# A fused attention and mixture-of-experts kernel: the chosen expert's second weights split in two halves around the state rows, part of expert 0's low parts made on GpSimd, its second load issued later

## The chip, the core and the metric

The kernel is one program on one core of a Trainium2 chip. The metric is the device time of a run in microseconds (us); the kernel before ran three times, 1128.51 to 1131.19 us, median 1130.11 us. Engines are named as in the profile: PE is TensorE, ACT is ScalarE, DVE is VectorE, POOL is GpSimd, SP is SyncE, which here only issues DMAs.

## What is computed

Three stages follow one another. Only the third, and the passage into it, is touched.

```python
xread, sread = two attentions between x (8 x 8 x 512 x 64) and state (8 x 8 x 32 x 64)
x = [xread, sread] as rows                     # 8 x 544 = 4352 rows of 512
h = x @ w_in; x = (h * clip(h + 3, 0, 6) / 6) @ w_out        # 512 -> 2048 -> 512
logits = x @ w_gate; e_idx = argmax(logits)    # 8 experts
for e in range(8):
    h  = max(x[e_idx == e] @ w1[e], 0)         # 512 -> 1024
    ye = h @ w2[e]                             # 1024 -> 512
    out[e_idx == e] = gate_w * sigmoid(x @ w_output_gate)[e] * ye
```

## The kernel before

Every product is made from two parts of each operand, a high part in fp32r (a copy made by ACT) and a low part (the operand less its high part, made by DVE), as three matmuls: high by high, high by low, low by high.

**The blocks.** Attention and the first MLP run over eight blocks of 512 rows, and then over one block B of the 256 state rows. After each block its rows are routed: the logits, the chosen expert, the place of each row among its expert's rows. POOL scatters the rows to `buckets` in HBM (`scatter_rows`, L757).

**The tiles of the expert stage.** The rows of an expert are worked in tiles of 128. Of tile t, `first` (L1014) multiplies the turned rows by the expert's first weights in two halves of 512 columns, `relu` (L1245, ACT) evicts a half, `hidden_out` (L656, SP) writes it to HBM and `hidden_back` (L663) reads it back in another layout, `turn_hidden` (L1626, DVE) and `hidden_hi` / `hidden_lo` (L1237 ACT, L1633 DVE) turn and split it, `second` (L1038) multiplies it by the second weights, `put_out` (L1616, DVE) scales it, and POOL scatters it to the output (L789). The rows of a tile come by `load_rows` (L640), `turn_rows` (L1604, DVE), `rows_hi` (L1218, ACT) and `rows_lo` (L1594, DVE).

**The weights.** An expert's first weights (2 MB) are loaded to `raw1`, the second weights (2 MB) to `raw2`, or for the first two experts to `raw2_first0` and `raw2_first1`. `split_hi` (L1210, ACT) and `split_lo` (L564, DVE) make high and low parts in four pieces of 128 x 1024. `w1_ready` and `w2_ready` count experts whose parts are all made; PE waits for them.

**The passage (PRE = 3 tiles).** After block 7 the fullest expert so far is chosen (`star`), and its first three tiles are worked while the state rows are still being routed. PE's order after the first MLP is: tile 0 first half, transposes of state rows 0 (`side(B + 1, 0)`), tile 0 second half, logits of state rows 0 and transposes 1, tile 1 first half, logits 1, tile 1 second half, tile 2 first half, ranks, tile 2 second half, the count of rows of all experts (L1052), then `second` of tiles 0, 1 and 2. From tile 3 on (expert 0, whose parts lie in the other weight slot) the order is `first(t)`, `second(t - 3)`.

**The table.** Meanwhile DVE computes from the counts which rows, expert and weight slot each of the 41 tiles has: a chain of small operations on 128 x 41 or 128 x 328 elements, each waiting for the one in front of it, from L1663 to L1749, with `turn_hidden`, `hidden_lo`, `put_out` and `turn_rows` of tiles 0 to 4 in between. `table_rows_ready` after L1688 lets SP load tile 3's rows; `order_ready` after L1722 is waited for by PE behind `first` of tile 3; `table_ready` after L1749 is waited for by ACT ahead of `relu` of tile 3 and by SP and POOL.

ACT, DVE, POOL and SP run what they are given in written order, so a wait holds whatever is written behind it on the same engine.

Of the kernel before, what the change touches and what calls it, by code (L numbers as in the profile page):

```python
# [29 lines left out]
ALU = mybir.AluOpType  # L30
# [9 lines left out]
def emit_kernel(nc, x_rows, x_t_dram, keys, w_in, w_out, gates, w1, w2, out):  # L40
# [30 lines left out]
    PRE = 3  # L71
# [144 lines left out]
    MT = MAX_TILES  # L216
# [90 lines left out]
    def sem(name):  # L307
        if name not in sems:
            sems[name] = nc.alloc_semaphore(name)
        return sems[name]  # L310
# [57 lines left out]
    def is_b(b, n):  # L368
        return isinstance(b, int) and b == n
# [164 lines left out]
    def by_pieces(raw):  # L534

        return raw[:].rearrange("p (i c) -> p i c", i=w1.shape[1])
# [38 lines left out]
    def _(sp):  # L575
# [134 lines left out]
        sp.wait_ge(sem("second_ready"), 1)  # L710
        e = sp.value_load(table[0:1, T_NEXT, MT:MT + 1], min_val=0, max_val=E - 1)
        sp.wait_ge(sem("w1_ready"), 2)
        sp.dma_start(by_pieces(raw1), w1[bass.ds(e, 1)].rearrange("o i p c -> p (o i) c")).then_inc(sem("raw1_loaded"), 16)
        load_rows(Tile(0, PRE + 2))

# [16 lines left out]
    def _(pool):  # L732
# [19 lines left out]
        def scatter_rows(b, tiles):  # L752

            wait(pool, "place_ready", b + 1)
            pool.sem_inc(sem("scatter_begun"), 1)
            for t in range(tiles):
                pool.indirect_dma_start(out=buckets, out_offset=bass.IndirectOffsetOnAxis(ap=place[:, t:t + 1], axis=0),  # L757
                                        in_=rows_of(b)[:, t, :], in_offset=None,
                                        bounds_check=limit, oob_is_err=False
                                        ).then_inc(sem("rows_stored"), 16)  # L760
# [18 lines left out]

        pool.wait_ge(sem("pads_stored"), 16 * (E + 1))  # L780

        scatter_rows(B, ST)

        def body(t):

            slot = t.slot
            wait(pool, "out_ready", t.n + 1)
            pool.sem_inc(sem("store_begun"), 1)
            pool.indirect_dma_start(out=out, out_offset=bass.IndirectOffsetOnAxis(ap=out_row[:, slot:slot + 1], axis=0),  # L789
                                    in_=yo_of(t)[:], in_offset=None, bounds_check=last_row, oob_is_err=False  # L790
                                    ).then_inc(sem(f"out_stored{slot}"), 16)

        for n in range(PRE):
            body(Tile(0, n))
        pool.wait_ge(sem("table_ready"), 1)
        stored = [pool.value_load(stores[0:1, s:s + 1], min_val=16 * (N_TOK // P // RING), max_val=16 * MT)
                  for s in range(RING)]
# [8 lines left out]
    def _(pe):  # L806
# [212 lines left out]
        def first(t):  # L1019

            expert, w_at = weights(t)
            wait(pe, "w1_ready", expert + 1)
            wait(pe, "xg_t_ready", t.n + 1)
            for h in range(HALVES):
                first_half(t, h, w_at)
# [46 lines left out]
    def _(act):  # L1072
# [167 lines left out]
        def relu(t, h):  # L1240
            wait(act, "hid2_ps", HALVES * t.n + h + 1)

            if h == 0:
                wait(act, "hid_written", 16 * HALVES * t.n)
            act.activation(expert_hid_of(t)[:, h * BANK:h * BANK + BANK], hid2_banks[t.slot % 2][:, h, :], ACT.Relu  # L1245
                           ).then_inc(sem("act_ready"), 1)

        side(B + 1, 0)
        relu(Tile(0, 0), 0)
        split_hi(1, 0, 0)  # L1250

        act.dma_start(by_pieces(raw2_first[1]), w2[0].rearrange("i p c -> p i c")).then_inc(sem("raw2_loaded"), 16)
        relu(Tile(0, 0), 1)
        side(B + 1, 1)
        rows_hi(Tile(0, 2))
        split_hi(0, 1, WSLOT, (0, 1))
        relu(Tile(0, 1), 0)
        side(B + 1, 2)
        split_hi(0, 1, WSLOT, (2, 3))
        relu(Tile(0, 1), 1)  # L1260
        hidden_hi(Tile(0, 0))
        relu(Tile(0, 2), 0)
        relu(Tile(0, 2), 1)
        hidden_hi(Tile(0, 1))
        split_hi(1, 1, WSLOT)
        hidden_hi(Tile(0, 2))
        rows_hi(Tile(0, 3))
        rows_hi(Tile(0, 4))
        act.wait_ge(sem("table_ready"), 1)
        act.wait_ge(sem("pads_stored"), 16 * (E + 1))  # L1270
# [53 lines left out]
    def _(dve):  # L1324
# [319 lines left out]
            mlp_block(b, S, CH)  # L1644
        mlp_block(B, NSB, ST)

        split_lo(dve, 1, 0, 0, signal="w2_ready")
        turn_rows(Tile(0, 2))
        side(B + 1, 1)
        rows_lo(Tile(0, 2))  # L1650
        split_lo(dve, 0, 1, WSLOT, (0, 1))
        side(B + 1, 2)
        split_lo(dve, 0, 1, WSLOT, (2, 3), "w1_ready")
        turn_hidden(Tile(0, 0))
        side(B + 1, 4)
        hidden_lo(Tile(0, 0))

        dve.wait_ge(sem("iota2"), 5)
        chain(dve.tensor_scalar(upto[:], upto[:], 0.0, None, ALU.is_ge))
        chain(dve.memset(t_chg[:, MT - 1:MT], 0.0))  # L1660
        dve.wait_ge(sem("count_ps"), 2)

        chain(dve.tensor_tensor(count[:], b_ps[:, 0, 0:E], star_sub[:], ALU.subtract))  # L1663
# [96 lines left out]
        def body(t):  # L1760
            split1 = split_code(dve, t)
            two_back = not (isinstance(t.n, int) and t.n < PRE + 2)
            if two_back:
                split2 = split_code(dve, t.plus(-2))
            split_first(t, split1)
            if not (isinstance(t.n, int) and t.n + 2 >= MT):
                turn_rows(t.plus(2))
                rows_lo(t.plus(2))
            if is_b(t.n, PRE):
                split_lo(dve, 1, 1, WSLOT, signal="w2_ready")  # L1770
            if two_back:
                with dve.If(split2 > 0):
                    split_lo(dve, 1, *next_of(split2), signal="w2_ready")
            if not is_b(t.n, PRE):
                turn_hidden(t.plus(-1))
                hidden_lo(t.plus(-1))
                if not (isinstance(t.n, int) and t.n < PRE + LAG2):
                    put_out(t.plus(-LAG2))
# [60 lines left out]
```

## Time and profile before

| | |
|---|---|
| runs | 1128.51, 1130.11, 1131.19 us |
| profiled execution | 1128.17 us, its span 1126.4 us |
| PE busy | 1104.0 us of the span, 6199 matmuls |
| DVE, ACT, POOL busy | 658.5, 476.6, 74.7 us |
| first MLP ends on PE | 685.2 us |
| tiles 0 to 2 on PE | 685.2 to 727.2 us |
| last result | 1126.4 us |

The span is the time from the first to the last instruction, 1.8 us less than the execution's own time. PE's busy time counts matmuls that overlap as one; what is left of the span is time in which PE had nothing that it was allowed to run.

### The profile page before, as it was taken

Reading aid. Unit: us, or ns where it says so; the run is one execution under the profiler, and the core shown is the slowest. Engines: PE = TensorE matmul, PEld = TensorE weight load, DVE = VectorE, ACT = ScalarE, POOL = GpSimd, SP = SyncE. Lnnn points to the kernel's source line nnn. Section 1 sums busy time; section 2 is a strip of 40 time slices with the busy share of each in tenths; the row PEclk is TensorE's granted clock in tenths of the full one; section 3 lists DMA queues with packets and bytes.
Section 4 is the critical chain, followed back from the end, with each engine's and each line's share of the span. In section 5 each row is a group of like instructions: output and inputs, shape, how many; then the busy total and the mean of one; then the engine's idle time right before and its main releaser. Section 6 shows DMA issues by size and latency. Waiting matters only on the chain.

```text
span 1126.4 us, 20220 instructions
## 1 busy us (share of the span) xinstructions
PE 1104.0 (98%) x6199; PEld 872.0 (77%) x6200; DVE 658.5 (58%) x1269; ACT 476.6 (42%) x789; POOL 74.7 (7%) x95
## 2 busy tenths in 40 slices
PE   9999999999999999999999999899999999999996
PEld 7777777777777777777777988677888888878885
DVE  6674665655655646646555455875665645558632
ACT  4454434434443443444354445343444333435320
POOL 0000100100101001001001010100011110101011
PEclk9999999999999999999999999999999999999999
DMA  9210211111102102111004079659877654785541
GB/s 364 106 39 1 76 39 38 38 39 38 43 33 75 38 1 76 38 38 40 1 1 132 1 260 285 197 174 284 263 240 232 218 173 139 234 258 181 168 154 60
DMA packets 129794, 135.59 MB, mean 120 GB/s; under 512 B 13999, under 2 KB 107823, under 8 KB 127152
## 3 DMA queue, kind: packets, MB, share of 16 engines
q1 hardware_dynamic: 95056, 87.26, 24.9%
q10 hardware_dynamic: 28896, 29.36, 8.3%
q0 software_dynamic: 5760, 17.90, 4.3%
q8 instruction: 49, 0.80, 0.3%
q14 instruction: 33, 0.27, 0.1%
HBM read 90.06 MB, written 45.47 MB: 120 GB/s over the span
## 4 chain that ended last, share of the span: by engine, by line
PE 87%; DVE 5%; DMA 2%; ACT 2%; issue 2%; SPq 1%; ACTq 1%; DVEq 0%; POOL 0%; POOLq 0%
PE y_ps L964 34%; PE h_ps L946 16%; PE y_ps L1038 15%; PE h_ps L1014 7%; PE y_ps L1014 6%; PE a_ps L921 3%; PE h_ps L936 2%; DMA hid_mv<-hidden 1%; DVE we L564 1%; ACT we L1210 1%; PE a_ps L819 1%; PE a_ps L905 1%; SPq L663 1%; PE a_ps L885 1%; PE b_ps L827 1%
## 5 line engine op out<-in xcount | busy, mean ns | idle before, releaser
L964 PE MATMUL y_ps<-w_out_hi,hid_hi 128*128 128x512 f32 x512 | 204.7, 400 | 0.0
L964 PE MATMUL y_ps<-w_out_hi,hid_lo 128*128 128x512 f32 x512 | 199.7, 390 | 0.0
L964 PE MATMUL y_ps<-w_out_lo,hid_hi 128*128 128x512 f32 x512 | 199.4, 389 | 0.0
L1038 PE MATMUL y_ps<-we,act_t_hi 128*128 (+1 forms) x608 | 188.5, 391 | 4.2 <-DVE yo L1616 2.2
L946 PE MATMUL h_ps<-att_hi,mix 128*128 128x512 f32 x512 | 184.1, 402 | 0.1
L1550 DVE SCALAR_TENSOR_TENSOR hid<-hid,h_ps 128x512 f32<-128x512 f32 x128 | 87.7, 685 | 144.9 <-ACT hid L1159 144.9
L1159 ACT ACTIVATE hid<-h_ps,three 128x512 f32<-128x512 f32 x128 | 87.9, 687 | 150.5 <-PE h_ps L946 150.4
L1038 PEld LDWEIGHTS y_ps<-we,act_t_hi 128*128 128x128 f32 x608 | 114.6, 189 | 28.9 <-issue 5.3
L964 PEld LDWEIGHTS y_ps<-w_out_hi,hid_hi 128*128 128x128 f32 x512 | 96.0, 188 | 49.1 <-issue 30.4
L1558 DVE TENSOR_TENSOR hid_lo<-hid,hid_hi 128x512 fp32r<-128x512 f32 x128 | 88.0, 687 | 62.8 <-ACT hid_hi L1166 62.3
L1038 PE MATMUL y_ps<-we,act_t_lo 128*128 (+1 forms) x304 | 118.7, 391 | 0.0
L946 PEld LDWEIGHTS h_ps<-att_hi,mix 128*128 128x128 f32 x512 | 96.1, 188 | 27.4 <-issue 7.0
L964 PEld LDWEIGHTS y_ps<-w_out_hi,hid_lo 128*128 128x128 f32 x512 | 96.1, 188 | 20.9
L964 PEld LDWEIGHTS y_ps<-w_out_lo,hid_hi 128*128 128x128 f32 x512 | 96.2, 188 | 18.8
L1166 ACT ACTIVATE hid_hi<-hid 128x512 fp32r<-128x512 f32 x128 | 80.7, 631 | 62.2 <-DVE hid L1550 59.9
L1237 ACT ACTIVATE act_t_hi<-act_raw 128x512 fp32r<-128x512 f32 x76 | 46.5, 632 | 129.2 <-DVE act_raw L1626 129.2
L946 PE MATMUL h_ps<-att_lo,mix 128*128 128x512 f32 x256 | 99.9, 390 | 0.0
L1014 PE MATMUL h_ps<-we,xg_t_hi 128*128 (+1 forms) x304 | 94.0, 390 | 2.5 <-DVE we L564 1.7
L1014 PE MATMUL y_ps<-we,xg_t_hi 128*128 (+1 forms) x304 | 94.1, 391 | 1.1 <-DVE xg_t_lo L1594 1.1
L1626 DVE STREAM_TRANSPOSE act_raw<-hid_mv 128x512 f32<-128x512 f32 x74 | 48.2, 689 | 60.4 <-DMA hid_mv<-hidden 30.6
L564 DVE TENSOR_TENSOR we<-raw,we 128x1024 f32 (+1 forms) x56 | 65.1, 1221 | 20.5 <-ACT we L1210 20.5
L757 POOL DMA_INDIRECT buckets<-rows,place x32 | 31.9, 998 | 594.9 <-DVE place L1496 587.6
(251 smaller groups left out, 1511.7 us busy)
## 6 DMA issues: line engine op xcount, KB each, us to landing
raw<-in_w ACTq DMA_DIRECT2D x12, 2048.0 KB, 10.6
hid_mv<-hidden SPq DMA_DIRECT2D x148, 128.0 KB
hidden<-expert_hid SPq DMA_DIRECT2D x70, 256.0 KB
xg<-buckets SPq DMA_DIRECT2D x156, 64.0 KB
xb<-in_x_rows SPq DMA_DIRECT2D x8, 1024.0 KB, 4.8
x_t<-in_x_t SPq DMA_DIRECT2D x7, 1024.0 KB, 4.9
buckets<-pad_row SPq DMA_DIRECT2D x8, 774.0 KB, 8.0
w_in_raw<-in_w_in SPq DMA_DIRECT2D x4, 1024.0 KB, 13.5
```

The lines of the kernel that those rows point to most:

```text
L564: ins = eng.tensor_tensor(we[:, bass.ds(w_at + piece(w, i, LO), PIECE)], raw[:, i * PIECE:(i + 1) * PIECE], we[:, bass.ds(w_at + piece(w, ...
L921: i = pe.matmul(mix_bank(a, n, g)[NS * q:NS * q + NS, :], keys_of(a)[D * g:D * g + D, q, :], w_in_raw[D * g:D * g + D, q, mix_columns(n)], ...
L946: i = pe.matmul(h_ps[:, j % 2, 0:cols], mix[:, m % SLOTS, g, n % GO, wp, :], (att1_hi, att1_lo)[tp][:, g, 0:cols], start=(g == 0 and k == ...
L964: i = pe.matmul(y_ps[:, t, :], hid_of(b, j)[1 + hp][:, t * P:(t + 1) * P], w_out_s[wp][:, j, :], start=(j == 0 and m == 0), stop=(j == KF ...
L1014: i = pe.matmul(hid2_banks[slot % 2][:, h, :], xg_t[xp][:, slot % 2, k, :], we[:, bass.ds(w_at + (wp * WPART + k * F + h * BANK), BANK)], ...
L1038: i = pe.matmul(y2_ps[:, slot % 2, :], act_t[hp][:, slot % 2, f, :], we[:, bass.ds(w_at + (wp * WPART + KD * F + f * DM), DM)], start=(f = ...
L1159: act.activation(whole, h_ps[:, j % 2, 0:cols], ACT.Relu, bias=three).then_inc(sem("relu_ready"), 1)
L1166: act.activation(high, whole, ACT.Copy).then_inc(sem("hid_hi_ready"), 1)
L1237: act.activation(act_t[HI][:, slot % 2, h * 4:h * 4 + 4, :], act_raw[:, slot % 2, h * 4:h * 4 + 4, :], ACT.Copy).then_inc(sem("act_t_hi"), 1)
L1550: dve.scalar_tensor_tensor(out=whole, in0=whole, scalar=6.0, in1=h_ps[:, j % 2, 0:cols], op0=ALU.min, op1=ALU.mult).then_inc(sem("swish_re ...
L1558: dve.tensor_tensor(low, whole, high.bitcast(F32), ALU.subtract).then_inc(sem("hid_ready"), 1)
L1626: dve.transpose(act_raw[:, slot % 2, h * 4:h * 4 + 4, :].rearrange("p f t -> p (f t)"), hid_mv_of(t)[:, h, :, :].rearrange("p s (k f) -> p ...
```

## The change

- ACT copies pieces 0 and 1 of the chosen expert's second weights ahead of the copy of the transposed state rows, and pieces 2 and 3 behind the first half's `relu` of tile 0; before, all four stood behind that `relu`.
- ACT issues the load of expert 0's second weights (`raw2_first1`, 2 MB) behind `relu` of tile 2; before, ahead of the second `relu` of tile 0.
- Pieces 2 and 3 of expert 0's first weights get their low parts from POOL (signal `w1_lo_pool`); PE waits for it ahead of tile 3, SP ahead of the next load into `raw1`.
- All four pieces of expert 0's second weights get their low parts from POOL, around its output scatters of tiles 0 to 2; before, DVE made them in tile 3's turn.
- ACT makes the high parts of these second weights in two halves around `rows_hi` of tile 3, behind `hidden_hi` of tile 2; before, all four ahead of `hidden_hi` of tile 2.
- DVE does two small operations of the table (`upto`, `t_chg`) before the passage. ACT does the second `relu` of tile 1 ahead of the last two `split_hi` pieces.

```diff
@@ sync, ahead of the load of the next first weights @@
         sp.wait_ge(sem("w1_ready"), 2)
+        sp.wait_ge(sem("w1_lo_pool"), 1)
@@ gpsimd @@
+        split_lo(pool, 0, 1, WSLOT, (2, 3), "w1_lo_pool")
         scatter_rows(B, ST)
...
-        for n in range(PRE):
-            body(Tile(0, n))
+        body(Tile(0, 0))
+        split_lo(pool, 1, 1, WSLOT, (0, 1, 2))
+        body(Tile(0, 1))
+        split_lo(pool, 1, 1, WSLOT, (3,), "w2_ready")
+        body(Tile(0, 2))
@@ tensor, first(t) @@
             wait(pe, "w1_ready", expert + 1)
+            if is_b(t.n, PRE):
+                pe.wait_ge(sem("w1_lo_pool"), 1)
@@ scalar @@
+        split_hi(1, 0, 0, (0, 1))
         side(B + 1, 0)
         relu(Tile(0, 0), 0)
-        split_hi(1, 0, 0)
-
-        act.dma_start(by_pieces(raw2_first[1]), w2[0].rearrange("i p c -> p i c")).then_inc(sem("raw2_loaded"), 16)
+        split_hi(1, 0, 0, (2, 3))
         relu(Tile(0, 0), 1)
         side(B + 1, 1)
         rows_hi(Tile(0, 2))
         split_hi(0, 1, WSLOT, (0, 1))
         relu(Tile(0, 1), 0)
         side(B + 1, 2)
+        relu(Tile(0, 1), 1)
         split_hi(0, 1, WSLOT, (2, 3))
-        relu(Tile(0, 1), 1)
         hidden_hi(Tile(0, 0))
         relu(Tile(0, 2), 0)
         relu(Tile(0, 2), 1)
+
+        act.dma_start(by_pieces(raw2_first[1]), w2[0].rearrange("i p c -> p i c")).then_inc(sem("raw2_loaded"), 16)
         hidden_hi(Tile(0, 1))
-        split_hi(1, 1, WSLOT)
         hidden_hi(Tile(0, 2))
+        split_hi(1, 1, WSLOT, (0, 1))
         rows_hi(Tile(0, 3))
+        split_hi(1, 1, WSLOT, (2, 3))
         rows_hi(Tile(0, 4))
@@ vector @@
+        dve.wait_ge(sem("iota2"), 5)
+        chain(dve.tensor_scalar(upto[:], upto[:], 0.0, None, ALU.is_ge))
+        chain(dve.memset(t_chg[:, MT - 1:MT], 0.0))
         split_lo(dve, 1, 0, 0, signal="w2_ready")
         turn_rows(Tile(0, 2))
         side(B + 1, 1)
         rows_lo(Tile(0, 2))
-        split_lo(dve, 0, 1, WSLOT, (0, 1))
+        split_lo(dve, 0, 1, WSLOT, (0, 1), "w1_ready")
         side(B + 1, 2)
-        split_lo(dve, 0, 1, WSLOT, (2, 3), "w1_ready")
...
-        dve.wait_ge(sem("iota2"), 5)
-        chain(dve.tensor_scalar(upto[:], upto[:], 0.0, None, ALU.is_ge))
-        chain(dve.memset(t_chg[:, MT - 1:MT], 0.0))
@@ vector, body(t) @@
-            if is_b(t.n, PRE):
-                split_lo(dve, 1, 1, WSLOT, signal="w2_ready")
```

What stands on POOL between its last constant and the wait for the table, before. `rows_state` are the 256 state rows, `yo` and `yo_pre` the results of tiles 0 to 2.

```order
L778 IOTA slot_back 128x4
L757 DMA buckets<-rows_state,place 38016x516 [waits pads_stored,place_ready]
L757 DMA buckets<-rows_state,place 38016x516
L789 DMA out<-yo_169,out_row 4352x512 [waits out_ready]
L789 DMA out<-yo_pre,out_row 4352x512 [waits out_ready]
L789 DMA out<-yo_169,out_row 4352x512 [waits out_ready]
```

The same place of the changed kernel. `raw_164` are expert 0's first weights, `raw_first_149` its second.

```order
L779 IOTA slot_back 128x4
L564 TENSOR_TENSOR we<-raw_164,we 128x1024 [waits w1_hi,pads_stored]
L564 TENSOR_TENSOR we<-raw_164,we 128x1024 [waits w1_hi]
L758 DMA buckets<-rows_state,place 38016x516 [waits place_ready]
L758 DMA buckets<-rows_state,place 38016x516
L792 DMA out<-yo_169,out_row 4352x512 [waits out_ready]
L564 TENSOR_TENSOR we<-raw_first_149,we 128x1024 [waits w2_hi] x3
L792 DMA out<-yo_pre,out_row 4352x512 [waits out_ready]
L564 TENSOR_TENSOR we<-raw_first_149,we 128x1024 [waits w2_hi]
L792 DMA out<-yo_169,out_row 4352x512 [waits out_ready]
```

Six subtractions with two inputs in SBUF now stand among POOL's scatters.

ACT at the beginning of the passage, before. `raw_first_148` are the chosen expert's second weights.

```order
L1180 ACTIVATE rows_state<-y_ps 128x512 [waits y_ps] x2
L1079 ACTIVATE rows_state_t<-a_ps 128x512 [waits t_ps]
L1245 ACTIVATE expert_hid_pre<-h_ps 128x512 [waits hid2_ps]
L1210 ACTIVATE we<-raw_first_148 128x1024 [waits raw2_loaded]
L1210 ACTIVATE we<-raw_first_148 128x1024 x3
L1252 DMA raw_first_149<-in_w 128x16x256
L1245 ACTIVATE expert_hid_pre<-h_ps 128x512 [waits hid2_ps]
```

The same place of the changed kernel.

```order
L1188 ACTIVATE rows_state<-y_ps 128x512 [waits y_ps] x2
L1218 ACTIVATE we<-raw_first_148 128x1024 [waits raw2_loaded]
L1218 ACTIVATE we<-raw_first_148 128x1024
L1087 ACTIVATE rows_state_t<-a_ps 128x512 [waits t_ps]
L1253 ACTIVATE expert_hid_pre<-h_ps 128x512 [waits hid2_ps]
L1218 ACTIVATE we<-raw_first_148 128x1024 [waits raw2_loaded]
L1218 ACTIVATE we<-raw_first_148 128x1024
L1253 ACTIVATE expert_hid_pre<-h_ps 128x512 [waits hid2_ps]
```

Two copies moved ahead of the transposed state rows, and the load left this place.

## Rows read from the trace of the kernel before

**Rows 1.** The page: busy time by engine.
```profile
PE 1104.0 (98%) x6199; PEld 872.0 (77%) x6200; DVE 658.5 (58%) x1269; ACT 476.6 (42%) x789; POOL 74.7 (7%) x95
```
**Rows 2.** PE's waits from 684 to 800 us: us, times, longest.
```profile
PE y_ps L1038 <- DVE yo L1616: 2.2, 1, 2.2
PE b_ps L1052 <- DVE seen L1499: 1.6, 1, 1.6
PE y_ps L1038 <- DVE act_t_lo L1633: 1.1, 1, 1.1
PE y_ps L1014 <- DVE xg_t_lo L1594: 1.1, 1, 1.1
PE h_ps L1014 <- issue: 0.9, 1, 0.9
PE y_ps L1038 <- issue: 0.8, 1, 0.8
PE b_ps L849 <- DVE logits L1331: 0.6, 1, 0.6
```
**Rows 3.** PE's timeline: start, us, instruction, idle before it; the count, tiles 0 and 7.
```profile
707.17 0.18 PE L1052 MATMUL b_ps<-seen,ones 128*128 128x8 bf16 x1 [1.63 <-DVE seen L1499]
708.46 1.19 PE L1038 MATMUL y_ps<-we,act_t_hi 128*128 128x512 f32 x2 [1.11 <-DVE act_t_lo L1633]
...
757.04 0.73 PE L1014 MATMUL y_ps<-we,xg_t_hi 128*128 x2 [1.05 <-DVE xg_t_lo L1594]
```
**Rows 4.** Windows: us, PE, PEld, DVE, ACT, POOL busy, granted PE clock, DMA.
```profile
708.00:710.00 2.00, 1.54 (x4) 1.28 (x5) 1.76 (x8) 0.00 (x0) 1.70 (x2) 0.50 0.69 198
```
**Rows 5.** ACT's timeline in the passage.
```profile
688.53 0.60 ACT L1079 ACTIVATE rows_state_t<-a_ps 128x512 f32<-128x512 f32 x1 [2.56 <-PE a_ps L819]
...
689.50 3.90 ACT L1210 ACTIVATE we<-raw_first 128x1024 fp32r<-128x1024 f32 x4
693.30 0.59 ACT L1245 ACTIVATE expert_hid_pre<-h_ps 128x512 f32<-128x512 f32 x1
```
**Rows 6.** SP's timeline: the hidden layer of tiles 0 and 2, out and back.
```profile
699.63 2.67 SPq L663 DMA_DIRECT2D hid_mv<-hidden  x4
...
708.69 1.01 SPq L656 DMA_DIRECT2D hidden<-expert_hid_pre  x2
713.57 2.53 SPq L663 DMA_DIRECT2D hid_mv<-hidden  x4
```
**Rows 7.** DMA queues from 693 to 699 us, ACT's: packets, MB, share of 16 engines.
```profile
q10 hardware_dynamic: 1538, 1.56, 78.2%
```
**Rows 8.** DVE's timeline from tile 2's hidden layer on.
```profile
718.97 1.31 DVE L1626 STREAM_TRANSPOSE act_raw<-hid_mv 128x512 f32<-128x512 f32 x2 [0.67 <-DMA hid_mv<-hidden]
...
734.26 0.18 DVE L1749 CAST table<-t_next 128x41 int32<-128x41 f32 x1
...
737.97 4.62 DVE L564 TENSOR_TENSOR we<-raw_first,we 128x1024 fp32r<-128x1024 f32 x4
...
745.98 1.30 DVE L1626 STREAM_TRANSPOSE act_raw<-hid_mv 128x512 f32<-128x512 f32 x2 [1.37 <-DMA hid_mv<-hidden]
...
769.66 1.30 DVE L1626 STREAM_TRANSPOSE act_raw<-hid_mv 128x512 f32<-128x512 f32 x2 [5.83 <-DMA hid_mv<-hidden]
```
**Rows 9.** The chain of waits: the write of tile 1's hidden layer: start, us, what.
```profile
704.02 2.01 DMA hidden<-expert_hid_pre
```
**Rows 10.** POOL's groups by shape: the only operation that reads SBUF elementwise.
```profile
L738 POOL TENSOR_SCALAR_AFFINE_SELECT ident<-ident 128x128 f32<-128x128 f32 x1 | 0.3, 288 | 0.3 <-POOL three L735 0.3
```
**Rows 11.** POOL's timeline: the two longest of its 72 scatters, and one beside them.
```profile
595.53 1.39 POOL L757 DMA_INDIRECT buckets<-rows,place  x1 [0.30 <-issue]
597.23 0.97 POOL L757 DMA_INDIRECT buckets<-rows,place  x1 [0.30 <-issue]
...
707.66 1.51 POOL L757 DMA_INDIRECT buckets<-rows_state,place  x1 [49.94 <-DVE place L1496]
```
**Rows 12.** A read-back of the hidden layer beside two loads of weights: its issue.
```profile
758.28 3.00 SPq L663 DMA_DIRECT2D hid_mv<-hidden  x4
```

## The prediction

> **What bounds it.** I read the page first: PE is busy for 1104.0 of 1126.4 us [rows 1]. The change adds and removes no matmul, so its reach is PE's 22 us without one. The table of PE's waits says where those lie that it can touch: 8.3 us in seven waits between 684 and 800 us, two behind results of the passage (`seen`, tile 0's `act_t_lo`), one behind tile 2's hidden layer (0.8), the others behind tiles 5 to 8 [rows 2]. To the first two a price belongs that no wait shows: from 708 to 710 us the granted clock is 0.50, the 1.2 GHz level, after PE had idled for 1.6 and 1.1 us with one small matmul between [rows 3, 4]. The first pair there takes 1.19 us [rows 3], the same pair 0.73 at the upper level [rows 3]; over the nine matmuls until the clock is back I estimate 1.4 us.
>
> Then I followed the other engines' timelines to see what sets the end of the stretch. Three things in a row do. (a) The hidden layers of tiles 0 to 2 go to HBM and back one after the other on SP; tile 2's is back at 718.97, DVE having waited 0.67 for it [rows 6, 8]. (b) From there DVE is never idle for long until the last table entry ends at 734.44, 15.5 us later [rows 8]. (c) ACT's `relu` of tile 3 waits for that table; tile 3's hidden layer is back at 745.98 [rows 8], behind it ACT and DVE split the next first weights, behind those stand tile 7's rows, and PE starts tile 7 at 757.04 [rows 3], 22.6 us behind the table. PE's waits of 1.1 and 2.2 us [rows 2] lie at the end of this sequence, not on matmuls. So **what counts is when the table is ready**; PE will idle until that plus 22.6 us whatever it gained earlier.
>
> **Part by part.** The sum is made against the profiled execution (span 1126.4, own time 1128.17 us), which is 1.9 us under the median 1130.11; I carry differences over unchanged.
>
> 1. Second weights in halves. ACT idled 2.56 us ahead of the state rows' copy [rows 5]; two of four copies at 0.98 us fit there, if the load has landed. On ACT's queue three loads of 2.1 MB pass from 676 to 699 us, 1.56 MB of them in its last 6 us [rows 7]; counting backwards the first is complete at about 685.4. The second `relu` of tile 0 then starts at 691.5 instead of 693.30 [rows 5], 1.8 us earlier. PE's 0.6 us wait for the logits goes too, since DVE's four subtractions end at 693 instead of 695.2.
>
> 2. The load leaves the queue. Behind the `relu` of 693.30 the read-back was issued only at 699.63 [rows 5, 6], 5.7 us after it ended, while ACT's queue moved its last 1.56 MB [rows 7]; for tile 1, with nothing beside it, it took 2.0 us [rows 9]. With the load gone I take 2.0: the read-back of tile 0 at 694.3, 5.3 us earlier, and tile 1's some 4 us earlier, near 702.3, set by PE's own pace.
>
> 3. Tile 2's hidden layer. PE ends tile 2 at 705.5 before [rows 3], at 704.7 now; its `relu` follows at once and SP is free: written from 705.2 instead of 708.69 [rows 6]. Now the moved load starts beside it (issue about 705.3), with the state rows' scatter. Undisturbed, the read-back would be in at 713.8; disturbed as the one issued at 758.28 [rows 12], which DVE got at 769.66 [rows 8] (11.4 us, where tile 2's took 5.4), at 720. A load of 2 MB beside it instead of the two there gives a third of that: 716.7, a gain of 2.3 us on 718.97 (ends: 5.2 and -1). DVE could not have used it before 714.6.
>
> 4. DVE's part of the first weights (two pieces, 2.3 us) leaves the passage. Tile 0's hidden layer is turned from 700.3, over 4 us earlier, ranks are placed by 702.8; without hindrance PE would go on from tile 2 to the count and tile 0's `second` at 704.8 instead of 708.46 [rows 3], at full clock. That is worth 3.7 + 1.4 us at that point, and nothing at the end, since PE then waits for tile 2 (716.7 + 2.7) and for (c).
>
> 5. `upto` and `t_chg` moved: 0.35 us off DVE, in front of a wait. Nothing.
>
> 6. DVE's 4.62 us of second weights at 737.97 [rows 8] go. Tile 6's rows are ready earlier and PE's 0.9 us wait [rows 2] disappears, but DVE had waited for tile 3's hidden layer at 745.98 anyway, so PE takes the 0.9 us again at tile 7. Nothing at the end.
>
> 7. What POOL does instead. No row shows a subtraction on POOL. From below: DVE's own 1.16 us a piece. The nearest row is the select of 128x128, 288 ns [rows 10], with one input: 2.25 ns a column, 2.3 us for 1024 columns; with every input costing that, 4.6. I take 2.3. Six pieces are 14 us on an engine that is 7% busy [rows 1]. The first two run from 701.2 to 705.8; the state rows' scatter behind them starts then, not later than 707.66 before [rows 11]. Three run behind the scatter of tile 0, from 720, when ACT has made their high parts (now behind tile 2's `hidden_hi`), one behind tile 1's. PE needs them at about 750, SP's added wait is over 15 us before its load, PE's added wait likewise. The output scatters of tiles 1 and 2 come later; nobody waits for them before 757. If POOL and DVE leave each other alone, all of it costs nothing.
>
> 8. **What POOL's subtractions do to DVE.** Two scatters of 72 are clearly longer than 0.97 us: 1.39 and 1.51, each while DVE ran a string of small operations in SBUF [rows 11]: 0.4 and 0.5 us of holding off, once each. Nothing shows the other direction with a POOL operation that reads two inputs. Bounds: none, or the whole of each piece in which DVE next meets an operation with two SBUF inputs (`rows_lo`, `used_no` at L1698, `over_mt` at L1714 and most steps of the table are such). With whole pieces: the piece at 720.0 holds `used_no` from 720.65 to 722.3 (1.65); the next takes hold as soon as that ends, 2.25; the third meets `over_mt` (0.75) and the fourth tile 4's `rows_lo` (0.9): 5.5 us between 718 and the last table entry. In the passage the first pair delays `seen` to 706.3 and tile 0's low part to 707.5, so that most of step 4 stays as it was, the low clock too. I take the whole: POOL's work is a piece at a time with no gap, and the string of table steps meets it everywhere.
>
> The Trainium skill, "SBUF — State Buffer", section "Who interferes with whom", says that a VectorE instruction with two SBUF inputs and a GpSimd one that reads SBUF exclude each other, the later one being fully blocked. By it step 8 is 5.5 us; by the scatters' 0.4 to 0.5 us a time four meetings would be 2. For the piece, "GPSIMD Engine Reference", section 3.1, has 4497 ns for 2048 columns; an estimate from it is 2.25 us.
>
> **Sum.** Table ready: -2.3 (step 3) + 5.5 (step 8) = +3.2 us, and from there the 22.6 us as before: 1130.1 + 3.2 = **1133.3 us**.
>
> **Rivals.**
> - *No holding off*: step 8 is nothing, the table is 2.3 to 3 us earlier, PE idles some 3 us ahead of tile 2's `second` and then follows. 1127.4 us, faster. For it: DVE's and POOL's other work beside each other shows 0.5 us at the most. Against: none of that work reads two inputs on POOL.
> - *Half of it*: holding off as in the scatters, or pieces that fall into DVE's one-input work (transposes, reductions); 2 to 2.5 us eat the gain of step 3. 1130.1 us, no change.
> - *The load collides*: no holding off, but tile 2's read-back is as slow as behind two loads, at 720 or later. The table is then 1 us later than before: 1131 us, at 722 slower by 3. It decides from 719 on.
> - *The halves don't fit*: if the first load lands after 687 us, `relu` of tile 0 and the state rows' copy slip by as much; each is covered by steps 2 and 3 up to 2 us. No case of its own.
>
> **Numbers.** A run of this kernel can tell 0.2%, 2.3 us, from no change. Whole holding off 0.44: slower 0.40, same 0.04. None 0.30: faster 0.24, same 0.06. Half 0.16: faster 0.04, same 0.10, slower 0.02. Collision 0.10: same 0.07, slower 0.03. So faster 0.28, same 0.27, slower 0.45. The likeliest case alone spans 1131.3 to 1135.5 (pieces of 1.7 to 3 us, step 3 by 1 us either way). Since the other sign has over a quarter, the range reaches from 1126.3 to 1135.5; below lies a gain of the whole 4.3 us that DVE leaves in step 3, above it a piece of 4.6 us.
>
> **What would show it.** Right: POOL's subtractions at 2.3 us or more; DVE's two-input steps of 0.2 us (`used_no`, `upto_n`, `over_mt`) shown as 1 to 2 us or with gaps of that size ahead of them; from tile 2's turned hidden layer to the last table entry 20 to 21 us instead of 15.5; PE's waits ahead of tiles 3, 4, 5 and 7. Read-back of tile 0 issued near 694 (step 2), tile 2's turned near 717 (step 3). Wrong: those 15.5 us unchanged or shorter (then the first rival), or tile 2 turned after 719 (the third). If PE's start of tile 7 moves by another amount than the last table entry does, (c) is wrong, and with it the sum.

## The result, and the profile after

Before and after ran by turns on one chip, five times each: median 1130.62 us before and **1141.13 us after** (1139.10 to 1144.35), ratio 1.0101, 95% interval 1.0083 to 1.0118. (The ratio is estimated from the single runs; the two medians lie 10.5 us apart, 0.9%.) The change costs some 10.5 us, where 3.2 were forecast; 1141.1 lies above the range, which ended at 1135.5. The profiled execution after has a span of 1139.3 us, 12.9 above that of before, whose own time (1128.17) was 2.4 us under its median.

PE of the kernel after, from 684 to 810 us, by what it waited for:

```profile
PE y_ps L1020 <- DVE xg_t_lo L1604: 4.4, 2, 2.8
PE y_ps L1046 <- issue: 3.2, 1, 3.2
PE b_ps L1060 <- DVE seen L1509: 2.5, 1, 2.5
PE y_ps L1046 <- DVE yo L1626: 2.5, 1, 2.5
PE h_ps L1020 <- issue: 1.9, 2, 1.7
PE y_ps L1046 <- DVE act_t_lo L1643: 1.1, 1, 1.1
PE y_ps L1020 <- issue: 0.8, 1, 0.8
```

16.4 us where [rows 2] had 8.3, and none is large: PE waits a little at nearly every tile, as an engine does that follows a late table. The rest of the 12.9 us is busy time: 4.7 us more for the same 6199 matmuls than in [rows 1], and the granted clock is under 1.00 behind some of these waits (the page, then the windows behind the wait of 2.8 us: busy time of PE, its weight load, DVE, ACT, POOL; granted clock, DMA share, GB/s):

```profile
PE 1108.7 (97%) x6199; PEld 875.4 (77%) x6200; DVE 662.9 (58%) x1263; ACT 476.3 (42%) x789; POOL 88.9 (8%) x101
```

```profile
730.00:735.00 5.00, 2.15 (x8) 1.47 (x7) 4.10 (x12) 2.52 (x3) 1.34 (x2) 0.89 0.17 43
735.00:740.00 5.00, 5.00 (x19) 4.00 (x18) 4.86 (x6) 0.63 (x1) 4.83 (x3) 0.77 1.08 361
```

So I follow the table again.

**POOL**, its subtractions and scatters, from 700 to 740 us (start, busy time of the group, how many; the bracket is the idle time ahead):

```profile
703.12 4.71 POOL L564 TENSOR_TENSOR we<-raw,we 128x1024 fp32r<-128x1024 f32 x2 [44.36 <-ACT we L1218]
...
720.98 0.97 POOL L792 DMA_INDIRECT out<-yo,out_row  x1 [9.52 <-DVE yo L1626]
725.65 4.76 POOL L564 TENSOR_TENSOR we<-raw_first,we 128x1024 fp32r<-128x1024 f32 x2 [3.71 <-ACT we L1218]
734.07 2.39 POOL L564 TENSOR_TENSOR we<-raw_first,we 128x1024 fp32r<-128x1024 f32 x1 [3.66 <-ACT we L1218]
736.61 0.99 POOL L792 DMA_INDIRECT out<-yo_pre,out_row  x1
737.62 2.40 POOL L564 TENSOR_TENSOR we<-raw_first,we 128x1024 fp32r<-128x1024 f32 x1
```

A piece takes 2.4 us; step 7 had 2.3. **DVE** beside these pieces (the first two rows from the passage, the rest from the table; the last is the last table entry):

```profile
703.61 1.95 DVE L1495 TENSOR_TENSOR place_f<-place_f,onehot 128x16 f32<-128x16 f32 x1
...
705.80 2.05 DVE L1506 CAST place<-g_best 128x2 int32<-128x2 f32 x1
...
722.65 1.31 DVE L1636 STREAM_TRANSPOSE act_raw<-hid_mv 128x512 f32<-128x512 f32 x2 [2.50 <-DMA hid_mv<-hidden]
...
725.73 2.37 DVE L1704 TENSOR_SCALAR table<-tile_no,total 128x41 int32<-128x41 f32 x1
728.13 2.31 DVE L1706 TENSOR_SCALAR used<-tiles_of 128x8 f32<-128x8 f32 x1
...
735.03 1.45 DVE L1719 TENSOR_SCALAR slot_n<-slot_back,total 128x4 int32<-128x4 f32 x1
...
737.78 2.29 DVE L1726 TENSOR_SCALAR t_left<-t_ord,nth 128x41 f32<-128x41 f32 x1
...
745.50 0.18 DVE L1758 CAST table<-t_next 128x41 int32<-128x41 f32 x1
```

Six operations that take 0.17 to 0.25 us in the kernel before stand for 1.45 to 2.37 us, each until a piece of POOL's ends (725.73 + 2.37 = 728.10, the middle of the pair; 728.13 + 2.31 = 730.44, its end). In the table they add 2.13 + 2.14 + 1.26 + 2.04 = 7.6 us. From tile 2's turned hidden layer (722.65) to the end of the last table entry (745.68) are 23.0 us, where [rows 8] had 15.5.

Its start is late too: 722.65 instead of 718.97 [rows 8]. 1.0 us of that I take as no work of the change: ACT's copy of the state rows, with which the passage begins and up to which the two programs differ by two small operations only (`upto` and `t_chg` on DVE, which then idles for 8.25 us), starts at 685.73 in this execution and at 684.69 in that of before (in the fourteen profiles of this case at 684.47 to 685.76). So 2.6 us are left. **ACT**, then **SP**, then the write of tile 2's hidden layer in the chain of waits (after, and the same of before), then the DMA queues from 706 to 718 us (packets, MB, the time their packets took as a share of 16 engines' span; q10 carries ACT's loads, q1 SP's transfers, q0 POOL's scatters):

```profile
688.82 2.01 ACT L1218 ACTIVATE we<-raw_first 128x1024 fp32r<-128x1024 f32 x2 [1.82 <-DMA raw_first<-in_w]
690.74 0.58 ACT L1087 ACTIVATE rows_state_t<-a_ps 128x512 f32<-128x512 f32 x1
...
693.58 0.60 ACT L1253 ACTIVATE expert_hid_pre<-h_ps 128x512 f32<-128x512 f32 x1
...
705.74 0.39 ACTq L1272 DMA_DIRECT2D raw_first<-in_w  x1
```

```profile
696.24 3.05 SPq L663 DMA_DIRECT2D hid_mv<-hidden  x4
...
706.71 1.21 SPq L656 DMA_DIRECT2D hidden<-expert_hid_pre  x2
717.73 2.54 SPq L663 DMA_DIRECT2D hid_mv<-hidden  x4
```

```profile
707.29 10.42 DMA hidden<-expert_hid_pre
```

```profile
709.27 4.28 DMA hidden<-expert_hid_pre
```

```profile
q10 hardware_dynamic: 2034, 2.07, 58.2%
q1 hardware_dynamic: 1180, 0.95, 26.3%
q0 software_dynamic: 160, 0.53, 11.0%
```

Tile 2's hidden layer is written from 706.71, 2.0 us earlier than before [rows 6], but its read-back is issued only at 717.73, 4.2 us later than before. Its 512 KB went out beside the moved load of 2 MB: the three queues fill 95.5% of those 12 us. It is the write that stood, 10.42 us instead of 4.28. The read-back was in 4.9 us after its issue (722.65), where it had been 5.4.

From the table to tile 7 all is as it was: PE starts tile 7 at 768.20, 22.5 us behind the end of the last table entry, where it had been 22.6. The `second` at 798.18 came at 786.75 before, with a wait of 2.19 instead of 2.48 us; after it the granted clock falls here and did not before. PE of the kernel after, then of before, then windows of the kernel after:

```profile
768.20 0.72 PE L1020 MATMUL y_ps<-we,xg_t_hi 128*128 x2 [1.55 <-DVE xg_t_lo L1604]
...
798.18 0.73 PE L1046 MATMUL y_ps<-we,act_t_hi 128*128 x2 [2.48 <-DVE yo L1626]
```

```profile
786.75 0.72 PE L1038 MATMUL y_ps<-we,act_t_hi 128*128 x2 [2.19 <-DVE yo L1616]
```

```profile
795.00:800.00 5.00, 2.52 (x10) 1.70 (x9) 3.52 (x7) 2.41 (x5) 0.97 (x1) 0.88 0.93 284
800.00:805.00 5.00, 5.00 (x19) 4.00 (x18) 3.92 (x7) 2.56 (x4) 0.00 (x0) 0.78 1.03 346
```

19 matmuls in 5 us instead of 24 at clock 1.00. So the 12.9 us of span are: 1.0 ahead of the passage, tile 2 turned 2.6 later, 7.6 us in the table (together the 11.2 by which tile 7 starts later), 0.3 more ahead of the `second` at 798.18, and an estimated 1.4 us of low clock behind it. Whether that low clock belongs to the change is not shown. Behind the same `second` the clock falls in e2, e6, e8 and e9 below too, and it stays at 1.00 in e4, after a wait of 2.6 us. This term and the 1.0 us at the start vary among the profiled executions whatever the edit, and the two medians lie 2.4 us less apart than the two spans.

### The profile page after: what moved, and what is told of

Read it like the earlier page. It is cut to its first block, busy times and chain, and to the rows that moved or that the text cites. A ratio compares the mean times of both kernels' runs of the same rounds, so it can differ in the third digit from the quotient of the medians.

```text
span 1139.3 us, 20223 instructions
## 1 busy us (share of the span) xinstructions
PE 1108.7 (97%) x6199; PEld 875.4 (77%) x6200; DVE 662.9 (58%) x1263; ACT 476.3 (42%) x789; POOL 88.9 (8%) x101
## 4 chain that ended last, share of the span: by engine, by line
PE 82%; DMA 5%; DVE 5%; issue 2%; ACT 2%; SPq 1%; ACTq 1%; DVEq 0%; POOL 0%; POOLq 0%
PE y_ps L970 32%; PE h_ps L952 16%; PE y_ps L1046 14%; PE h_ps L1020 6%; PE y_ps L1020 6%; PE a_ps L927 3%; DMA raw<-in_w 2%; PE h_ps L942 2%; DMA raw_first<-in_w 1%; DMA hid_mv<-hidden 1%; DVE we L564 1%; DMA hidden<-expert_hid_pre 1%; ACT we L1218 1%; PE a_ps L911 1%; PE a_ps L825 1%
## 5 line engine op out<-in xcount | busy, mean ns | idle before, releaser
L564 DVE TENSOR_TENSOR we<-raw,we 128x1024 f32 (+1 forms) x54 | 62.7, 1222 | 20.6 <-ACT we L1218 20.6
```

The costliest lines, as they stand in the source:

```text
L564: ins = eng.tensor_tensor(we[:, bass.ds(w_at + piece(w, i, LO), PIECE)], raw[:, i * PIECE:(i + 1) * PIECE], we[:, bass.ds(w_at + piece(w, ...
```

## The experiments

Two theories at first. **Both together**: POOL's pieces hold off the table by 7.6 us, the moved load delays tile 2 by 2.6 us, and the sum goes through to the end. **One hidden by the other**: one of the two alone explains the time and the other would be covered. Later ones asked which operations POOL holds off, and whether the load has a place that costs nothing. "Start" is where ACT begins to copy the state rows, "tile 2" how long after it DVE starts to turn tile 2's hidden layer, "table" how long after it the last table entry ends, all in the profiled execution; the stretch lies between the last two. The ratio is the estimate from the single runs, as above; it differs from the quotient of the medians by up to 0.1%.

| kernel | median us (before beside it) | ratio, 95% interval | start | tile 2 | table | stretch |
|---|---|---|---|---|---|---|
| before | 1130.11 |  | 684.69 | 34.3 | 49.8 | 15.5 |
| after | 1141.13 (1130.62) | 1.0101, 1.0083 to 1.0118 | 685.73 | 36.9 | 59.9 | 23.0 |
| e1_load_back | 1134.64 (1129.99) | 1.0047, 1.0030 to 1.0064 | 685.64 | 32.6 | 55.6 | 23.0 |
| e2_no_pool | 1132.88 (1129.99) | 1.0026, 1.0015 to 1.0036 | 684.52 | 37.2 | 52.7 | 15.5 |
| e3_pool_second_only | 1137.39 (1129.99) | 1.0076, 1.0057 to 1.0094 | 685.20 | 34.1 | 58.2 | 24.1 |
| e4_load_only | 1136.01 (1129.99) | 1.0064, 1.0045 to 1.0082 | 684.69 | 40.5 | 55.9 | 15.5 |
| e5_halves_only | 1129.31 (1129.38) | 0.9992, 0.9983 to 1.0001 | 684.47 | 33.9 | 49.4 | 15.5 |
| e6_load_after_tile2 | 1130.38 (1129.38) | 1.0004, 0.9994 to 1.0014 | 684.69 | 31.0 | 50.1 | 19.1 |
| e7_pieces_apart | 1137.20 (1129.38) | 1.0066, 1.0051 to 1.0082 | 685.76 | 33.8 | 57.8 | 24.0 |
| e8_load_after_rows3 | 1133.97 (1130.18) | 1.0032, 1.0021 to 1.0043 | 685.70 | 31.2 | 46.6 | 15.5 |
| e9_rows5_first | 1129.06 (1129.20) | 0.9997, 0.9988 to 1.0006 | 685.24 | 32.1 | 47.6 | 15.5 |
| p2_pool_subtracts, one run | 1132.44 (1129.38) |  | 684.54 | 34.1 | 53.9 | 19.7 |
| p3_pool_memsets, one run | 1127.61 (1130.18) |  | 684.61 | 33.5 | 49.7 | 16.2 |
| p4_pool_copies, one run | 1129.80 (1130.18) |  | 685.37 | 34.1 | 50.5 | 16.4 |

In most of them the time follows the table's column within some 1 us: after +10.2 there and +10.5 in the median, e1 +5.9 and +4.7, e2 +3.0 and +2.9, e3 +8.4 and +7.4, e4 +6.2 and +6.0, e5 -0.3 and -0.1, e6 +0.3 and +1.0, e7 +8.1 and +7.8. In e8 (-3.1 and +3.8) and e9 (-2.1 and -0.1) it does not; there something behind the table is late.

### One part undone

e1_load_back is the kernel after with the load at its old place:

```diff
@@ ACT, before relu(Tile(0, 0), 1)
+        act.dma_start(by_pieces(raw2_first[1]), w2[0].rearrange("i p c -> p i c")).then_inc(sem("raw2_loaded"), 16)
@@ ACT, behind relu(Tile(0, 2), 1)
-        act.dma_start(by_pieces(raw2_first[1]), w2[0].rearrange("i p c -> p i c")).then_inc(sem("raw2_loaded"), 16)
```

> The changed kernel with the load of expert 0's second weights back at its old place, ahead of tile 0's second relu. Theory: two costs add up in the change, the moved load beside tile 2's way through HBM (tile 2's hidden layer was turned at 722.65 instead of 718.97, 3.7 us) and GpSimd's subtractions holding VectorE (7.5 us from there to the last table entry). Then tile 2 is turned near 719, the stretch to the last entry stays about 23 us, and the time is 1141.1 - 3.7 = 1137.4 us. Rival: tile 2 is late because the state rows' scatter stands behind GpSimd's first two pieces; then nothing moves, 1141 us.

Measured 1134.64, 4.65 over its before where after has 10.51: undoing the load's move gives 5.9 us, not the 3.7 expected. Tile 2, and the table with it, come 4.3 us earlier than there, with the state rows' scatter still behind POOL's first two pieces: the rival falls. The other 1.6 us lie behind the table: the `second` that waited 2.48 us at 798.18 waits 0.61 here, and the clock stays at 1.00 behind it (it falls to 0.71 behind tile 7 instead). That they come with the load's place is not shown: e4 has the load moved and takes no longer than before from its table to the end, and each of the two medians is known to some 2 us only.

e2_no_pool is the kernel after with all six pieces made by DVE in their old places; the load and the halves stay moved:

```diff
@@ POOL
-        split_lo(pool, 0, 1, WSLOT, (2, 3), "w1_lo_pool")
...
-        split_lo(pool, 1, 1, WSLOT, (0, 1, 2))
...
-        split_lo(pool, 1, 1, WSLOT, (3,), "w2_ready")
@@ DVE, at the places of before; PE and SP no longer wait for w1_lo_pool
+        split_lo(dve, 0, 1, WSLOT, (2, 3), "w1_ready")
...
+        split_lo(dve, 1, 1, WSLOT, signal="w2_ready")
```

> The changed kernel with all six pieces made on VectorE at the places of the kernel before, no other difference: the load stays moved, the halves stay. Theory: the 7.5 us of held VectorE instructions go, the late tile 2 stays: stretch from tile 2's turn to the last entry 15.5 us, tile 2 near 722, 1141.1 - 7.5 = 1133.6 us. Rival (VectorE is slow in the table for another reason, such as DMA traffic beside it): stretch 23 us, 1141 us or more.

Measured 1132.88, 0.7 under the 1133.6 expected. The stretch is 15.5 us again, and tile 2 is 3.0 us later than before: the load's collision stays, with no piece of POOL's anywhere, and the hold-off is gone.

Do the two parts add? Against e5 below, which has neither, the last table entry is 3.3 us later in e2, 6.2 in e1 and 10.5 with both, 1.0 more than their sum. Over their befores the medians are 2.9 and 4.7 us, and 10.5 with both: 2.9 more than the sum, but each is uncertain by 1 to 2 us. So they add, and whether some 1 to 3 us come on top is not settled.

### One part alone

e3_pool_second_only is the kernel before with the second weights' four pieces on POOL; e4_load_only the kernel before with the load moved; e5_halves_only the kernel after without POOL's pieces and with the load back, so that only ACT's halves and order and DVE's early `upto` remain.

> The kernel before with only the four low parts of expert 0's second weights moved to GpSimd, between its output scatters; ScalarE's order and the load as before. Theory: three or four VectorE instructions of the table are held for up to 2.4 us each, last entry 6 to 8 us later, 1130.6 + 5.5 to 7.5 = 1136 to 1138 us. Rival (holding costs only beside the other edits; the 4.6 us taken off VectorE pay for it): within 1 us of 1130.6.

e3: 1137.39, 7.4 us slower, as expected. POOL's row, then DVE's:

```profile
720.47 6.97 POOL L564 TENSOR_TENSOR we<-raw_first,we 128x1024 fp32r<-128x1024 f32 x3
```

```profile
720.68 7.92 DVE L1636 TENSOR_TENSOR act_t_lo<-act_raw,act_t_hi 128x512 fp32r<-128x512 f32 x2
...
735.51 2.27 DVE L1720 TENSOR_SCALAR t_left<-t_ord,nth 128x41 f32<-128x41 f32 x1
```

The first of the two `act_t_lo` stands 7.3 us, through all three pieces, the second takes its usual 0.68. Tile 2's `second` waits on PE for 7.0 us behind it.

> The kernel before with only the load of expert 0's second weights moved behind tile 2's relu. Theory: the load runs beside tile 1's and tile 2's hidden layers, tile 2 is turned 3 to 4 us later than 718.97 and everything with it: 1130.6 + 3.7 = 1134.3 us. Rival (the load costs nothing at either place, as a read-back issued earlier makes up for it): 1130 us.

e4: 1136.01, 1.7 over the 1134.3 expected. Here ACT's order is the old one, and the load, issued at 706.33, meets tile 1's read-back as well:

```profile
706.04 2.65 SPq L663 DMA_DIRECT2D hid_mv_pre<-hidden  x4
708.80 1.01 SPq L656 DMA_DIRECT2D hidden<-expert_hid_pre  x2
719.86 2.53 SPq L663 DMA_DIRECT2D hid_mv<-hidden  x4
```

```profile
717.82 1.30 DVE L1625 STREAM_TRANSPOSE act_raw<-hid_mv_pre 128x512 f32<-128x512 f32 x2 [7.42 <-DMA hid_mv_pre<-hidden]
```

Again 11 us from the write of tile 2's hidden layer to its read-back; both tiles are late, tile 2 by 6.2 us, and the time follows.

> The kernel before with ScalarE's halves and order and the two early table operations of the change; all pieces on VectorE, the load at its old place. Theory (load and GpSimd are the whole of the loss): tile 0's second relu is 0.5 to 1.8 us earlier but the table is bound by tile 2's hidden layer at about 718.5, so 1129.0 to 1130.0 us, no more than 1 us under the kernel before. Rival (the halves cost by themselves, since ScalarE waits for the first load ahead of the state rows): 1131 to 1132 us.

e5: no difference, as expected. ACT waited 1.8 us for the first load here too, so the halves could not bring all that step 1 wanted.

### What POOL holds off

e7_pieces_apart is e3 with a wait behind each of the first three pieces, so that they don't follow each other at once; p2, p3 and p4 are the kernel before with other work on POOL behind tile 0's scatter, on a buffer that nobody reads any more, with a wait behind each. The three ran once each, so their rows are read and not their times.

```diff
+        ...                      # spare_t: rows_state_t as 128x512
+        for i in range(6):       # p3: 12 x memset; p4: 12 x tensor_copy of 128x256
+            pool.tensor_tensor(spare_t, spare_t, spare_t, ALU.subtract).then_inc(sem("probe"), 1)
+            pool.wait_ge(sem("probe"), i + 1)
```

> The kernel with only expert 0's second weights on GpSimd, with a wait for each of the first three pieces' completion ahead of the next. In the run without the waits one VectorE subtraction of 128x512 stood for 7.3 us, as long as three pieces. Theory (pieces that follow with no gap keep VectorE's two-input instruction out until the last is done): with the gap the instruction gets in between two pieces, lasts 2 to 2.5 us, and the time falls by 2 to 4 us from 1137.4. Rival (a gap makes no difference): 7 us and 1137 us again.

e7: 1137.20, as slow as e3; the 2 to 4 us did not come, though the operation got in between two pieces. The two `act_t_lo` now take 3.11 and 2.82 us instead of 7.32 and 0.68, and next in line a TENSOR_SCALAR of 0.24 stands 2.17: what one operation is spared the next ones pay. A TENSOR_SCALAR of 128x1 between them kept its 0.14 with the third piece running.

> The kernel before with six extra GpSimd subtractions of 128x512 (two inputs in SBUF) behind tile 0's scatter, each waited for; they work on a tile that nobody reads any more. Theory: each is 1.2 us; VectorE's two-input and SBUF-to-SBUF one-input instructions among them stand up to 1.2 us longer, three to five of them; transposes and reductions keep their 0.7 and 0.2 us. Rival: nothing is held by instructions this short.

p2: DVE's `act_t_lo` took 1.48 and 1.52 us, two TENSOR_SCALAR of the table 0.84 and 1.09, `used_no` (two inputs) 0.89; reductions kept their times, as expected. No transpose lay beside these; in the kernel after one that began at 734.41, beside a piece, took its usual 0.70. The stretch grew by 4.3 us.

> The kernel before, with twelve memsets of 128x512 on GpSimd behind the scatter of tile 0's outputs, one after the other with a gap between them (they fill rows_state_t, which nobody reads any more). They write SBUF and read nothing. In p2_pool_subtracts six subtractions of 1.24 us there, with gaps, made tile 2's two act_t_lo 1.48 and 1.52 us long (0.69 alone), two TENSOR_SCALAR of the table 0.84 and 1.09, used_no 0.89. Theory (the Trainium skill's rule, the page SBUF - State Buffer): a two-input VectorE instruction is held off only by a GpSimd instruction that reads SBUF, a one-input one (TENSOR_SCALAR, CAST) by any. By it act_t_lo stay at 0.69 to 0.75 and used_no at 0.2, while some of the TENSOR_SCALAR of 0.14 to 0.2 us (total, table, used) stand at 0.4 us or more. Rival: whatever GpSimd does holds off both sorts; then act_t_lo take 1.0 us or more. Second rival: only GpSimd's two inputs hold anything off; then all stand as in the kernel before.

p3, POOL and then DVE:

```profile
719.90 7.02 POOL L797 MEMSET rows_state_t<- 128x512 f32 x12
```

```profile
719.57 1.29 DVE L1639 TENSOR_TENSOR act_t_lo<-act_raw,act_t_hi 128x512 fp32r<-128x512 f32 x2
...
721.24 0.47 DVE L1701 TENSOR_SCALAR table<-tile_no,total 128x41 int32<-128x41 f32 x1
721.74 0.53 DVE L1703 TENSOR_SCALAR used<-tiles_of 128x8 f32<-128x8 f32 x1
722.31 0.17 DVE L1704 TENSOR_TENSOR used_no<-used,expert_no 128x8 f32<-128x8 f32 x1
```

Beside a writer that reads nothing, both `act_t_lo` and `used_no` keep their times, and TENSOR_SCALAR of 0.24 and 0.17 us stand until a memset of 0.53 ends. The theory's line between the two sorts holds in this execution.

> The same with twelve copies of 128x256 on GpSimd in place of the memsets (one SBUF input, one output). Theory (the skill's rule): both sorts of VectorE instruction are held off, as in p2_pool_subtracts: act_t_lo at 0.9 us or more (0.69 alone) and one or more of the TENSOR_SCALAR of the table and used_no at 0.4 us or more. Rival: only GpSimd instructions with two inputs hold VectorE off; then act_t_lo stay under 0.8 and all small ones under 0.3.

p4: with one input on POOL the two `act_t_lo` take 1.77 us together instead of 1.29, the same two TENSOR_SCALAR 0.38 and 0.41, but `used_no` 0.17 and `upto_n` 0.31. `act_t_lo` is just short of the 0.9 each that was written down; the direction is the theory's, since beside memsets of longer duration they did not move at all. POOL is held too: one of its twelve copies took 0.83 us instead of 0.40.

The Trainium skill, "SBUF — State Buffer", section "Who interferes with whom", says both halves of this: a VectorE instruction with two SBUF inputs contends with a GpSimd instruction that reads SBUF, not with one that only writes it; and a copy, cast or `tensor_scalar` within SBUF can run in a mode that contends with GpSimd. p3 agrees with the first (`act_t_lo` 1.29 us for two beside memsets), and with the second p3 (0.47 and 0.53) and the four TENSOR_SCALAR of the kernel after (1.45 to 2.37 us).

### Where the load could go

All three have DVE make all low parts (e2) and the halves of the chosen expert's weights. The load's place differs, and with it that of expert 0's second high parts; e9 moves tile 5's rows as well.

```diff
@@ e6, ACT: the load behind hidden_hi(Tile(0, 2)), the four high parts behind rows_hi(Tile(0, 4))
@@ e8, ACT: the load one line further down, behind rows_hi(Tile(0, 3))
@@ e9, as e8, and SP
-        load_rows(Tile(0, PRE + 2))      # was behind the load of the next first weights
         sp.wait_ge(sem("second_ready"), 1)
+        load_rows(Tile(0, PRE + 2))      # now ahead of it
@@ e9, ACT: split_hi(1, 1, WSLOT) in tile 3's turn, behind rows_hi of tile 5
```

> As the run without GpSimd's pieces, with the load of expert 0's second weights issued behind tile 2's hidden layer (near 717 us) and its high parts behind tile 4's rows. Theory: no hidden layer of tiles 0 to 2 has a load beside it; tile 2 is turned near 715 to 716 instead of 718.97, the last table entry is 2.5 to 3.5 us earlier than 734.4, 1127 to 1128 us, faster than both kernels. Rival: the load now meets tile 3's rows and the next first weights, ScalarE's four copies stand ahead of tile 3's relu: 1131 us or more.

e6: 1130.38, no difference; the forecast gain did not come, and tile 3's rows, which the rival named, took it, though not to the rival's 1131. Tile 2 is turned at 715.66, 3.3 us earlier than before, so the gain of step 3 exists; DVE does not wait for it there, its own work sets this start. DVE then stands for tile 3's rows:

```profile
715.66 1.29 DVE L1627 STREAM_TRANSPOSE act_raw<-hid_mv 128x512 f32<-128x512 f32 x2
...
723.98 0.71 DVE L1605 STREAM_TRANSPOSE xg_raw<-xg 128x512 f32<-128x512 f32 x1 [3.49 <-DMA xg<-buckets]
```

> e6_load_after_tile2 with one line moved: the load of expert 0's second weights is issued behind tile 3's rows_hi, some 7 us later, instead of behind tile 2's hidden_hi. In e6 the table was late because tile 3's rows came 3.5 us late beside the load, though tile 2 was turned 3.3 us earlier than in the kernel before. Theory (the load costs what it collides with): tile 2 is turned near 715.7 as in e6, tile 3's rows are no longer waited for by more than 0.5 us, the last table entry ends at 731 to 732 instead of 734.4, and the time is 1127 to 1128 us. Rival: the load then runs beside the next first weights and tile 4's rows, and the second weights are ready only after 750; then PE waits for tile 4's rows or the second weights, and the time is 1130 us or more.

e8: 1133.97, 3.8 us slower, where 1127 to 1128 were expected. The table ends 3.1 us earlier than before, counted from the start, as the theory said; then DVE waits 6.1 us for tile 5's rows, which stand behind two loads of 2 MB:

```profile
739.48 0.71 DVE L1605 STREAM_TRANSPOSE xg_raw<-xg 128x512 f32<-128x512 f32 x1 [6.08 <-DMA xg<-buckets]
```

```profile
PE y_ps L1015 <- DVE xg_t_lo L1595: 6.0, 1, 6.0
```

> e8_load_after_rows3 with two things moved: SP issues tile 5's rows ahead of the next first weights instead of behind them, and ACT makes expert 0's second high parts behind tile 3's relu and tile 5's rows_hi instead of ahead of them. In e8 the last table entry ended at 732.3, 2.3 us earlier than in the kernel before, but two loads of 2 MB lay in front of tile 5's rows, DVE waited 6.1 us for them at 739.5 and PE as much at 742.2; and ACT's split waited 10.2 us for its load with tile 3's relu behind it. Theory (each load costs what stands behind it): the last table entry again at 732 to 733, tile 5's rows turned at 734 or before, tile 7 started by PE at 755 to 756 instead of 757.04, and the time 1127.5 to 1129 us, a little under the kernel before. Rival: with two loads in the air until 736 or later the second weights are split too late, or tile 3's hidden layer is as slow beside them as tile 2's was in the changed kernel (10 us for its write); then PE starts tile 7 at 757 or later and the time is 1130 us or more.

e9: 1129.06, no difference. The table ends 2.1 us earlier, but tile 3's hidden layer is turned at 746.42 (745.98 before) and PE starts tile 7 at 757.48 (757.04 before; 755 to 756 expected): counted from the start both are where they were, and the 2.1 us are gone. None of the three places gave a gain, and no version here beats the kernel before.

## Why the prediction was wrong

Its sign came out and one of its two mechanisms (slower was the likeliest case, by POOL holding off DVE); what it said of tile 2's way through HBM did not, and so the size did not: +3.2 forecast, +10.5 measured. Of the 7.3 us between them step 3 has 4.9 and step 8 has 2.1.

- **Step 1, failed.** "Counting backwards the first is complete at about 685.4": ACT still waited 1.82 us for it at 688.82, and the second `relu` came at 693.58 (692.5 less the 1.0 us of the start) instead of 691.5. The 685.4 follows from no row: an even division of the 23 us among three loads gives 683.7, and the load was in later than either. Little hung on it, as the case without a chance of its own said; e5 shows the halves at nothing.
- **Step 2, nearly right.** The read-back of tile 0 was issued at 696.24, 4.4 us earlier than before counted from the start; 5.3 were forecast.
- **Step 3, failed, 4.9 us of the miss.** It was to gain 2.3 us and lost 2.6 (722.65, or 721.6 less the start's 1.0, against 716.7). The step put the collision on the read-back, at a third of what one had lost beside two loads. (That third, 2.1 us, gives 716.7 from the 714.6 before which DVE could not use it; from the 713.8 of the text it gives 715.9.) But the read-back took no longer than before, 4.9 us; the write ahead of it, for which the step had no delay, stood: 11.0 us from its issue to the read-back's instead of 4.9, beside one load of 2 MB issued 1.0 us ahead of it. The bound on the other side (720) was passed as well. e6 shows that without the load the gain is there, 3.3 us and not the 5.2 of the other bound, since DVE has no time for it earlier.
- **Steps 4 to 6, as said for the end.** PE had no gain in the passage: `seen` was held by POOL's first pair, and PE's count at 708.17 is, less the 1.0 us of the start, where it was before [rows 3]; of DVE's removed 4.6 us nothing showed.
- **Step 7, right.** 2.3 forecast, 2.4 measured.
- **Step 8, right in kind, 2.1 us too small.** 7.6 instead of 5.5. It counted only DVE operations with two SBUF inputs. What stood were four TENSOR_SCALAR (and a CAST in the passage), which it took for safe: p3 shows why. Four meetings were forecast and four there were, three of them for 2.0 us or more of a 2.4 us piece; beside a subtraction on POOL either sort is held (p2), so nearly every step that comes next can be.
- **(c), right.** 22.5 us from the table to tile 7, against 22.6.
- **What no step had**: the low clock at 798, an estimated 1.4 us in the profiled execution, not shown to be the change's.
- **The rivals** "the load collides" and "POOL holds off" were given as alternatives with a chance each, and the range reached to each alone. They happened together; e1 and e2 show each without the other. With its own 722 for tile 2 (+3) and 5.5 for the hold-off the text would have given +8.5.

## What to carry to other kernels

Work moved from VectorE to GpSimd is not off VectorE's path: while GpSimd ran an operation of 2.4 us in SBUF, a step of VectorE's of 0.2 us stood until it ended, four times in one table, so a serial string of small steps is a bad neighbour. (Pieces put behind such a string were not tried here.) A large load that leaves one queue arrives beside something else: list the small transfers with a waiter in the 10 us behind its new place, writes too, and price each as nearly as long as the load (here 10.4 us for 512 KB instead of 4.3). When two rivals do not exclude each other, one case has to be both.

## What the runs showed of the hardware that was not expected

- A VectorE TENSOR_SCALAR of 128 x 4 to 128 x 41 in SBUF (0.17 to 0.25 us alone) stands until GpSimd's operation is over, also beside a memset (0.47 and 0.53 beside memsets of 0.53). One of 128 x 1 did not stand (0.14 in e7, with a piece running). Nor did every larger one: one of 128 x 8 kept its 0.17 in p2, where it began within 0.1 us of the start of a subtraction of GpSimd's.
- Three GpSimd subtractions back to back kept a 128 x 512 subtraction of VectorE out for 7.32 us (e3), while in the kernel after the small `place_f` with two SBUF inputs got in between the two of a pair (1.95 us), and so did a TENSOR_SCALAR (2.37 us). What decides whether an operation gets in at the seam was not settled.
- From the issue of tile 2's write (512 KB) to that of its read-back 11.0, 11.3 and 11.1 us passed beside a 2 MB load (after, e2, e4), and 4.9, 5.7 and 2.7 without one (before, e5, e6).
